# Attention streamed between the matmuls of a dense layer: pooled scores moved to columns of their own, into one insertion with the local scores, one slot later

## The chip, the cores and the metric

The kernel runs on one core of a Trainium2 chip. The engines are PE (TensorE, matmul), DVE (VectorE), ACT (ScalarE), POOL (GpSimd) and SP, which issues most of the DMAs. Each has its own instruction queue and runs it in order; semaphores tie them together. The metric is the time of one execution on the device in microseconds (us); lower is better. The median of three runs of the kernel before is 809.03 us (808.3 to 810.23).

## The reference, what matters

```python
# q, k, v: (4 batches, 8 heads, 576 positions, 64), fp32
q_d = q.reshape(B, H, 144, 4, 64).mean(axis=3)        # likewise k_d, v_d
out_d = softmax(scale * q_d @ k_d.T) @ v_d            # pooled attention, 144 x 144
out_up = np.repeat(out_d, 4, axis=2)
mask = abs(i - j) < 4                                 # local attention, a band of 7 keys
out_local = softmax(where(mask, scale * q @ k.T, -1e9)) @ v
x = (out_up + out_local) as (2304 tokens, 512)
h = x @ w_in;  x = (h * clip(h + 3, 0, 6) / 6) @ w_out          # d_ff 2048
h = max(x @ w1, x @ w2, x @ w3);  out = h @ w_out2              # d_ff 768
```

## The kernel before, in words

Attention is done for two heads at a time, a *pair*; there are 16 pairs, four to a batch (`PAIRS` = 4). Pairs 0 to 3 are done in a prologue, before the dense layers, with their instructions in an order written by hand. Pairs 4 to 15 are the *streamed* pairs: their instructions are put between the matmuls of the first dense layer, which makes PE the engine that has work all the time.

The first dense layer runs over 5 chunks of tokens (512 wide, the last one 256) and 16 slices of d_ff: 80 steps. Every product is made of three matmuls on high and low parts (`three`, L686 to L690). In step s, PE issues, in this order: `hidden(s + 1)`, the 12 matmuls of the first product for the next step; the even slot 2s; `add_out(s)`, the 12 matmuls of the second product; the odd slot 2s + 1. The hidden value goes through ACT (`gate_relu`, L1100), DVE (`gate`, L1384), ACT (`gate_high`, L1106) and DVE (`gate_low`, L1391); `add_out` waits for the last of them. `hidden(s)` waits until `gate(s - 1)` has emptied the one bank that it writes.

A *slot* is the place at which each engine puts in its part of a streamed pair (`attend`). `FIRST` (L145) gives the slot in which a pair starts: 0, 7, 14 and 21 for pairs 4 to 7, and 30, 38, 46 and so on to 86 for pairs 8 to 15. Pairs 5 and 7 so start in an odd slot, the others in an even one. `STAGES` (L146) gives how many slots later each stage comes:

- stage 0: PE transposes q and k (`turn_q`, `turn_k`), ACT copies them out (`copy_q`, `copy_k`, which count `s_cqk`), DVE sums them by fours (`pool_qk`), POOL sums v (`sum_v`).
- stage 1: PE makes the local scores (`scores_local`, L745, 20 products of 64 x 64, shown as 40 instructions) in columns 0 to 319 of the two banks `ba` and `bb`. DVE adds the mask (L1265), takes the maximum (L1273) and subtracts it (L1280).
- stage 2: PE makes the pooled scores (`scores_down`, L762, four products of 72 x 144, shown as 8 instructions) in columns 0 to 287 of the same two banks, once the mask has been added, that is once the local scores have been read. ACT takes the exponentials (`exp_local` L1024, `exp_down` L1033), DVE the pooled maximum (`max_down` L1309) and the local sum and its inverse (L1317 to L1323), POOL multiplies the local part (`norm_local`, L623).
- stage 2 plus one slot: DVE makes the inverse of the pooled sums (`inverse_down`, L1329, L1331), and POOL multiplies the pooled part by it (`norm_down`, L633).
- stage 3 (slot 5): PE transposes the local part (`turn_local`, L775) and then the pooled part (`turn_down`, L789), which waits for `norm_down`.
- stage 4 (slot 6): PE multiplies with v (L800, L823), and DVE adds both parts up into x (`put_x`, L1347).

In the first chunk the weights are split as well: ACT copies slice s + 3 (`high_w1`, L1072) right after `gate_high(s + 1)` and before the odd slot, and POOL subtracts (`low_w1`, L641). POOL's order in step s is: even slot 2s, `low_w1(s + 3)`, odd slot 2s + 1. The last slice, 15, is split in step 12. In steps 0 and 1 PE has no `hidden` of its own, since the prologue has done it; so nothing lies between slots 1 and 2 there.

DVE's order in step s is: `gate(s + 1)`, slot 2s, `gate_low(s + 1)`, slot 2s + 1. ACT's is: `gate_relu(s + 1)`, slot 2s, `gate_high(s + 1)`, `high_w1(s + 3)`, slot 2s + 1.

Of the kernel before, what the change touches and what calls it, by code (L numbers as in the profile page):

```python
# [7 lines left out]
ACT = mybir.ActivationFunctionType  # L8
# [53 lines left out]
def attention_moe_kernel(  # L62
# [18 lines left out]
    PAIRS = H // 2  # L81
# [8 lines left out]
    KW = 64  # L90
    QW = 58
    NT = 10
    TPH = NT // 2
# [7 lines left out]
    def tile_of(h, x, t):  # L101

        upper = (t + h) % 2
        return upper * LOWER[h] + 2 * (t // 2) + x
# [12 lines left out]
    SD = S // FACTOR  # L117
    DT = SD // 2
# [24 lines left out]

    FIRST = {4: 0, 5: 7, 6: 14, 7: 21, 8: 30, 9: 38, 10: 46, 11: 54, 12: 62, 13: 70, 14: 78, 15: 86}  # L145
    STAGES = (0, 1, 2, 5, 6)  # L146

    def at_slot(slot):

        return [(n, slot - a) for n, a in FIRST.items() if 0 <= slot - a <= STAGES[4]]  # L150

# [7 lines left out]
    def splits_of(slot):  # L159
        found = [EARLY[slot]] if slot in EARLY else []  # L160
        late = [(n // PAIRS, n // PAIRS, n % PAIRS) for n, a in FIRST.items() if slot == a + STAGES[4]]
        return found, late
# [56 lines left out]
    with ExitStack() as ctx:  # L219
# [4 lines left out]
        def sem(name):  # L224
            return ctx.enter_context(nc.semaphore(name))
# [61 lines left out]
        def tiles(n):  # L287
            return work_b if n == 1 else work_c if n == 2 else work_a
# [44 lines left out]
        s_cqk = sem("s_cqk")  # L333
        s_pool = sem("s_pool")
        s_sl = sem("s_sl")
        s_madd = sem("s_madd")
# [8 lines left out]
        s_dmax = sem("s_dmax")  # L345
# [218 lines left out]
        def _(pool):  # L564
# [35 lines left out]
            def sum_v(n):  # L600
                to, t = land(n), tiles(n)

                pool.wait_ge(to.s_v4, 32 * turn_of(n))
                g.tensor_tensor(to.v4[:, :, :, 0:2, :].rearrange("r t h j d -> r (t h) (j d)"),
                                to.v4[:, :, :, 0:2, :].rearrange("r t h j d -> r (t h) (j d)"),
                                to.v4[:, :, :, 2:4, :].rearrange("r t h j d -> r (t h) (j d)"),
                                ALU.add).then_inc(s_vpart, 1)
                pool.wait_ge(s_vpart, n + 1)
                if before(n) >= 0:

                    pool.wait_ge(s_pvd, before(n) + 1)
                g.tensor_tensor(t.vd[:].rearrange("r t (h d) -> r (t h) d", h=2),
                                to.v4[:, :, :, 0, :].rearrange("r t h d -> r (t h) d"),
                                to.v4[:, :, :, 1, :].rearrange("r t h d -> r (t h) d"),
                                ALU.add).then_inc(s_vd, 1)
# [30 lines left out]
            def attend(slot):  # L646
                for n, i in at_slot(slot):
                    if i == STAGES[0]:
                        sum_v(n)
                    if i == STAGES[2]:  # L650
                        norm_local(n)
                    if i == STAGES[2] + 1:
                        norm_down(n)
# [29 lines left out]
        def _(pe):  # L683
            mm = nc.tensor.matmul
# [41 lines left out]
            def scores_local(n):  # L726
                t = tiles(n)

                pe.wait_ge(s_cqk, 4 * n + 4)
                if n < PAIRS:  # L730

                    pe.wait_ge(s_mb, 1)
                    pe.wait_ge(s_idb, 1)
                    for x in range(2):
                        for h, dst in enumerate((t.ba, t.bb)):
                            rows = slice(h * KW, (h + 1) * KW)
                            mm(dst[x * KW:(x + 1) * KW, 0:TPH * KW], identb[rows, rows],
                               maskb[rows, x].rearrange("p t w -> p (t w)"), start=True, stop=False,
                               skip_group_check=True)
                for i in range(TPH):  # L740
                    for x in range(2):
                        for h, dst in enumerate((t.ba, t.bb)):
                            a = QW * tile_of(h, x, i)
                            rows = slice(h * D, (h + 1) * D)
                            mine = mm(dst[x * KW:(x + 1) * KW, i * KW:(i + 1) * KW], t.qT[rows, a:a + KW],  # L745
                                      t.kT[rows, a:a + KW], start=n >= PAIRS, stop=True, skip_group_check=True)
                mine.then_inc(s_sl, 1)

            def scores_down(n):
                t = tiles(n)  # L750

                pe.wait_ge(s_pool, 2 * n + 2)

                if n < PAIRS:
                    pe.wait_ge(s_lsub, n + 1)
                else:
                    pe.wait_ge(s_madd, 2 * (n - PAIRS) + 2)
                for i in range(2):
                    for h, dst in enumerate((t.ba, t.bb)):  # L760
                        rows = slice(h * D, (h + 1) * D)
                        mine = mm(dst[0:DT, i * SD:(i + 1) * SD], t.qd[rows, i * DT:(i + 1) * DT],  # L762
                                  t.kd[rows, :], start=True, stop=True)
                mine.then_inc(s_sd, 1)

            def turn_local(n):
# [61 lines left out]
            def attend(slot):  # L828
                for n, i in at_slot(slot):
                    if i == STAGES[0]:  # L830
                        turn_q(n)
                        turn_k(n)
                    if i == STAGES[1]:
                        scores_local(n)
                    if i == STAGES[2]:
                        scores_down(n)
                    if i == STAGES[3]:
                        turn_local(n)
                        turn_down(n)
                    if i == STAGES[4]:  # L840
                        values_down(n)
                        values_local(n)
# [157 lines left out]
        def _(act):  # L1000
            fn = nc.scalar.activation
# [24 lines left out]
            def exp_down(n):  # L1026
                t = tiles(n)

                act.wait_ge(s_dmax, 2 * n + 2)
                for h, src in enumerate((t.ba, t.bb)):  # L1030
                    for i in range(2):
                        at = 2 * h + i
                        mine = fn(t.dp[:, h, i, :], src[0:DT, i * SD:(i + 1) * SD], ACT.Exp,  # L1033
                                  bias=t.dnm[:, at:at + 1], accum_out=t.dsum[:, at, 0:1])
                mine.then_inc(s_dexp, 1)

# [209 lines left out]
        def _(dve):  # L1246
            vec = nc.vector
# [56 lines left out]
            def max_down(n):  # L1304
                t = tiles(n)

                dve.wait_ge(s_sd, n + 1)
                for h, src in enumerate((t.ba, t.bb)):
                    vec.tensor_reduce(t.dnm[:, 2 * h:2 * h + 2],  # L1309
                                      src[0:DT, 0:2 * SD].rearrange("p (t w) -> p t w", w=SD),  # L1310
                                      AX, ALU.max, negate=True).then_inc(s_dmax, 1)

            def inverse_local(n):
# [96 lines left out]
            for t in (work_a, work_b, work_c):  # L1410
# [4 lines left out]
                mine = vec.memset(t.qT[:, S:], 0.0)  # L1415
# [97 lines left out]
```

## Time and profile before

| | |
|---|---|
| median of three runs | 809.03 us |
| the profiled execution, its own time | 810.8 us |
| its span, first to last instruction | 809.0 us |
| PE matmul, busy | 793.4 us, 98% of the span |
| DVE, ACT, POOL, busy | 314.1, 277.3, 164.1 us |
| mean granted TensorE clock | 0.998 |
| the chain that ended last, share on PE | 93% |

How to read it: the two pieces of work that set the time are the matmuls themselves and the moments at which PE has none to issue. A row of the timeline is one group of instructions: its start, its length, the engine, line and operation, and in square brackets how long the engine was idle before it. Matmuls overlap in the pipeline, so the distance between two starts tells more than a length: undisturbed, the matmuls of the dense layer start about 0.23 us apart. The granted clock is at its upper level, 2.4 GHz, in all of the stretches that matter here.

### The profile page before, as it was taken

What the parts mean: (1) busy time and instruction counts of PE and PEld (TensorE: products, weight loads), DVE (VectorE), ACT (ScalarE), POOL (GpSimd) and SP (SyncE); (2) the same over time, 40 slices, a digit from 0 to 9 for tenths busy, and PEclk for the clock granted to TensorE, in tenths of its full rate; (3) what the DMA queues carried; (4) which work ended last, traced back from release to release, by engine and by line L of the source; (5) the groups of instructions that cost most, each with busy time, mean ns of one, the idle gap of its engine ahead of it and who ended that gap; (6) DMA issues with size and microseconds to landing.
All of it is one profiled execution on the core that took longest, in us unless ns stands there. A gap on an engine that the chain in (4) does not pass through costs nothing.

```text
span 809.0 us, 12700 instructions
## 1 busy us (share of the span) xinstructions
PE 793.4 (98%) x5344; PEld 659.0 (81%) x5344; DVE 314.1 (39%) x602; ACT 277.3 (34%) x619; POOL 164.1 (20%) x196
## 2 busy tenths in 40 slices
PE   7889999999999999999999999999999999999998
PEld 5667877888787878788888899888888888888897
DVE  5864556355444554553323334232123123112211
ACT  4745555343343434433223256221112112111111
POOL 7855756221022102210000048100000000000000
PEclk9999999999999999999999999999999999999999
DMA  8982412221211321110200066100110020010010
GB/s 176 207 260 69 113 48 61 57 79 39 62 39 32 103 62 32 30 32 30 76 1 0 1 196 188 61 0 1 53 52 1 36 70 0 14 66 0 14 40 27
DMA packets 93477, 49.06 MB, mean 61 GB/s; under 512 B 61164, under 2 KB 84204, under 8 KB 93420
## 3 DMA queue, kind: packets, MB, share of 16 engines
q1 hardware_dynamic: 90740, 47.36, 21.3%
q10 hardware_dynamic: 2680, 0.89, 0.6%
q8 instruction: 42, 0.69, 0.4%
q14 instruction: 15, 0.12, 0.1%
HBM read 38.79 MB, written 9.44 MB: 60 GB/s over the span
## 4 chain that ended last, share of the span: by engine, by line
PE 93%; POOL 2%; DVE 2%; ACT 1%; DMA 1%; SPq 1%; issue 1%; DVEq 0%; POOLq 0%
PE bank L688 29%; PE bank L690 28%; PE bank L689 28%; PE bank L823 1%; PE bank L800 1%; PE bank L745 1%; PE bank L789 1%; PE bank L762 1%; DMA k_nat_c<-in_k_dram 1%; PE bank L775 1%; POOL w L641 1%; PE bank L707 1%; POOL dp_a L633 1%; PE bank L717 1%; SPq L415 0%
## 5 line engine op out<-in xcount | busy, mean ns | idle before, releaser
L688 PE MATMUL bank<-xs,w 128*128 128x512 f32 (+1 forms) x680 | 253.5, 373 | 1.1 <-DVE xs L1356 1.0
L689 PE MATMUL bank<-xs,w 128*128 128x512 f32 (+1 forms) x680 | 250.5, 368 | 0.0
L690 PE MATMUL bank<-xs,w 128*128 128x512 f32 (+1 forms) x680 | 250.4, 368 | 0.0
L688 PEld LDWEIGHTS bank<-xs,w 128*128 128x128 f32 x680 | 128.4, 189 | 23.4 <-POOL w L641 1.4
L690 PEld LDWEIGHTS bank<-xs,w 128*128 128x128 f32 x680 | 128.3, 189 | 21.7
L689 PEld LDWEIGHTS bank<-xs,w 128*128 128x128 f32 x680 | 128.4, 189 | 20.4
L688 PE MATMUL bank<-gs,w 128*128 128x512 f32 (+1 forms) x320 | 121.6, 380 | 0.0
L1384 DVE SCALAR_TENSOR_TENSOR rg<-rg,bank 128x512 f32<-128x512 f32 (+1 forms) x80 | 50.7, 634 | 177.3 <-ACT rg L1100 177.3
L689 PE MATMUL bank<-gs,w 128*128 128x512 f32 (+1 forms) x320 | 118.1, 369 | 0.0
L690 PE MATMUL bank<-gs,w 128*128 128x512 f32 (+1 forms) x320 | 118.0, 369 | 0.0
L1100 ACT ACTIVATE rg<-bank,half 128x512 f32<-128x512 f32 (+1 forms) x80 | 51.6, 646 | 177.8 <-PE bank L690 177.8
L1391 DVE TENSOR_TENSOR gs<-rg,gs 128x512 fp32r<-128x512 f32 (+1 forms) x80 | 61.6, 770 | 39.2 <-ACT gs L1106 39.1
L1474 DVE TENSOR_TENSOR hm<-hm,bank 128x512 f32<-128x512 f32 (+1 forms) x30 | 19.0, 635 | 136.9 <-ACT hm L1215 136.9
L688 PEld LDWEIGHTS bank<-gs,w 128*128 128x128 f32 x320 | 60.3, 188 | 12.0 <-issue 1.9
L690 PEld LDWEIGHTS bank<-gs,w 128*128 128x128 f32 x320 | 60.3, 189 | 10.5
L689 PEld LDWEIGHTS bank<-gs,w 128*128 128x128 f32 x320 | 60.4, 189 | 8.9
L1215 ACT ACTIVATE hm<-bank 128x512 f32<-128x512 f32 (+1 forms) x30 | 16.7, 555 | 140.1 <-PE bank L690 140.1
L1106 ACT ACTIVATE gs<-rg 128x512 fp32r<-128x512 f32 (+1 forms) x80 | 47.3, 591 | 31.3 <-DVE rg L1384 31.3
L641 POOL TENSOR_TENSOR w<-w_raw,w 128x256 fp32r<-128x256 f32 x64 | 47.2, 768 | 28.4 <-ACT w L1072 28.4
L678 POOL TENSOR_TENSOR w<-w_raw,w 128x1024 fp32r<-128x1024 f32 x12 | 28.9, 2411 | 116.3 <-ACT w L1128 116.3
L1479 DVE TENSOR_TENSOR hs<-hm,hs 128x512 fp32r<-128x512 f32 (+1 forms) x30 | 19.2, 639 | 79.4 <-ACT hs L1223 79.4
L623 POOL TENSOR_TENSOR lp_a<-lp_a,linv_a 128x320 f32<-128x320 f32 x28 | 20.2, 741 | 145.8 <-DVE linv_a L1323 145.8
(211 smaller groups left out, 822.5 us busy)
## 6 DMA issues: line engine op xcount, KB each, us to landing
w_raw<-in_moe_w_out_dram SPq DMA_DIRECT2D x22, 256.0 KB, 4.8
w_raw<-in_moe_w_dram SPq DMA_DIRECT2D x18, 256.0 KB, 3.2
out_dram<-o_sb SPq DMA_DIRECT2D x18, 256.0 KB, 2.0
w_raw<-in_moe_w_in_dram SPq DMA_DIRECT2D x16, 256.0 KB, 3.9
x_scratch<-y SPq DMA_DIRECT2D x4, 1024.0 KB, 4.8
xr<-x_scratch SPq DMA_DIRECT2D x4, 1024.0 KB, 6.4
q_nat_a<-in_q_dram SPq DMA_DIRECT2D x26, 144.0 KB, 2.8
v_a<-in_v_dram SPq DMA_DIRECT2D x24, 144.0 KB
```

Source lines behind the costliest of these rows:

```text
L623: mine = g.tensor_tensor(lp[:, a:b], lp[:, a:b], t.linv[:, a:b].unsqueeze(2).to_broadcast([P, b - a, KW]), ALU.mult)
L641: mine = g.tensor_tensor(w1[:, f, 1, 2 * i:2 * i + 2], w1_raw[f][:, 2 * i:2 * i + 2], w1[:, f, 0, 2 * i:2 * i + 2].bitcast(F32), ALU.subtract)
L678: g.tensor_tensor(w2[:, m, 1], w2_raw[m][:], w2[:, m, 0].bitcast(F32), ALU.subtract).then_inc(s_w2, 1)
L688: mm(dst, w[0], m[0], start=start, stop=False, skip_group_check=True)
L689: mm(dst, w[0], m[1], start=False, stop=False, skip_group_check=True)
L690: return mm(dst, w[1], m[0], start=False, stop=stop, skip_group_check=True)
L1100: fn(gated(s), hidden_bank(s)[:, 0:n], ACT.Relu, bias=half[:, 0:1], scale=1.0 / 6.0).then_inc(s_relu, 1)
L1106: fn(gs[:, s % 2, 0, 0:n], gated(s), ACT.Copy).then_inc(s_gh, 1)
L1384: vec.scalar_tensor_tensor(out=gated(s), in0=gated(s), scalar=1.0, in1=hidden_bank(s)[:, 0:n], op0=ALU.min, op1=ALU.mult).then_inc(s_g, 1)
L1391: vec.tensor_tensor(gs[:, s % 2, 1, 0:n], gated(s), gs[:, s % 2, 0, 0:n].bitcast(F32), ALU.subtract).then_inc(s_gl, 1)
L1474: vec.tensor_tensor(got, got, bank[HBANK[f % 2][1]][:, 0:n], ALU.max).then_inc(s_m1, 1)
L1479: vec.tensor_tensor(hs[:, f, 1, 0:n], got, hs[:, f, 0, 0:n].bitcast(F32), ALU.subtract).then_inc(s_hl, 1)
```

## The change

`STAGES` goes from (0, 1, 2, 5, 6) to (0, 2, 3, 5, 6). In a streamed pair nothing is done in slot 1 any more. In slot 2 PE makes first the pooled scores and then the local scores; the pooled ones get columns that the local ones do not use, by the new function `pooled`: two of the four products go to a third bank (`bc`), one to `bb` and one to `ba` from column 320 on. `scores_down` no longer waits for the mask to be added. The work of DVE on the local scores moves to slot 2; the exponentials, `max_down`, `inverse_local` and `norm_local` move to slot 3; `inverse_down` and `norm_down` move to slot 4. The transposes stay in slot 5. `max_down` has three reductions in place of two. For the pairs of the prologue everything stays as it was.

```diff
-    STAGES = (0, 1, 2, 5, 6)
+    STAGES = (0, 2, 3, 5, 6)
+
+    def pooled(n, t, at):
+        if n < PAIRS:
+            return (t.ba, t.bb)[at // 2][0:DT, at % 2 * SD:(at % 2 + 1) * SD]
+        if at < 2:
+            return t.bc[0:DT, at * SD:(at + 1) * SD]
+        return (t.bb, t.ba)[at - 2][0:DT, TPH * KW:TPH * KW + SD]
...
# scores_down, PE
                 if n < PAIRS:
                     pe.wait_ge(s_lsub, n + 1)
                 else:
-                    pe.wait_ge(s_madd, 2 * (n - PAIRS) + 2)
+                    pe.wait_ge(s_cqk, 4 * n + 4)
                 for i in range(2):
-                    for h, dst in enumerate((t.ba, t.bb)):
+                    for h in range(2):
                         rows = slice(h * D, (h + 1) * D)
-                        mine = mm(dst[0:DT, i * SD:(i + 1) * SD], t.qd[rows, i * DT:(i + 1) * DT],
-                                  t.kd[rows, :], start=True, stop=True)
+                        mine = mm(pooled(n, t, 2 * h + i), t.qd[rows, i * DT:(i + 1) * DT],
+                                  t.kd[rows, :], start=True, stop=True, skip_group_check=True)
...
# attend, PE
                     if i == STAGES[1]:
+                        scores_down(n)
                         scores_local(n)
-                    if i == STAGES[2]:
-                        scores_down(n)
...
# exp_down, ACT
-                act.wait_ge(s_dmax, 2 * n + 2)
+                act.wait_ge(s_dmax, 2 * n + 2 + max(0, n - PAIRS + 1))
...
-                        mine = fn(t.dp[:, h, i, :], src[0:DT, i * SD:(i + 1) * SD], ACT.Exp,
+                        mine = fn(t.dp[:, h, i, :], pooled(n, t, at), ACT.Exp,
...
# max_down, DVE
+                parts = ((t.ba, 0, 0, 2), (t.bb, 0, 2, 4))
+                if n >= PAIRS:
+                    parts = ((t.bc, 0, 0, 2), (t.bb, TPH * KW, 2, 3), (t.ba, TPH * KW, 3, 4))
+                for src, first, a, b in parts:
+                    vec.tensor_reduce(t.dnm[:, a:b],
+                                      src[0:DT, first:first + (b - a) * SD].rearrange("p (t w) -> p t w", w=SD),
                                       AX, ALU.max, negate=True).then_inc(s_dmax, 1)
```

## Rows read from the trace of the kernel before

**Rows 1.** The page, busy time of each engine (share of the span, instructions).

```profile
PE 793.4 (98%) x5344; PEld 659.0 (81%) x5344; DVE 314.1 (39%) x602; ACT 277.3 (34%) x619; POOL 164.1 (20%) x196
```

**Rows 2.** Who waited for whom: total us, times, longest us.

```profile
PE bank L789 <- POOL dp_a L633: 1.6, 3, 0.8
PE bank L762 <- DVE lp_a L1265: 1.1, 1, 1.1
```

**Rows 3.** Timeline of PE, pair 9 (start, length, group).

```profile
188.24 0.39 PE L690 MATMUL bank<-gs,w 128*128 128x512 f32 x1
188.56 0.81 PE L745 MATMUL bank<-kT_a,qT_a 64*64 64x64 f32 x40
189.30 0.50 PE L688 MATMUL bank<-xs,w 128*128 128x512 f32 x1
...
191.93 0.39 PE L690 MATMUL bank<-xs,w 128*128 128x512 f32 x1
192.25 0.71 PE L762 MATMUL bank<-kd_a,qd_a 64*72 64x144 f32 x8
192.89 0.50 PE L688 MATMUL bank<-gs,w 128*128 128x512 f32 x1
...
195.74 0.39 PE L688 MATMUL bank<-xs,w 128*128 128x512 f32 x1
...
198.24 0.39 PE L690 MATMUL bank<-xs,w 128*128 128x512 f32 x1
...
201.19 0.71 PE L775 MATMUL bank<-ident,lp_a 128*128 128x128 f32 x5
201.73 0.67 PE L789 MATMUL bank<-ident,dp_a 72*72 72x72 f32 x8
```

**Rows 4.** Timeline of DVE and ACT, pair 9.

```profile
189.44 0.89 DVE L1265 TENSOR_TENSOR lp_a<-bank,mask 128x320 f32<-128x320 f32 x2 [0.83 <-PE bank L745]
...
191.22 0.82 DVE L1280 TENSOR_TENSOR lp_a<-lp_a,lnm_a 128x640 f32<-128x640 f32 x1
...
192.35 0.69 ACT L1100 ACTIVATE rg<-bank,half 128x512 f32<-128x512 f32 x1 [4.67 <-PE bank L690]
...
193.68 0.81 DVE L1309 TENSOR_REDUCE dnm_a<-bank 72x2 f32<-72x288 f32 x2
...
195.25 0.17 DVE L1321 TENSOR_REDUCE leps_a<-lsum_a 128x10 f32<-128x20 f32 x1
...
195.46 0.22 DVE L1323 RECIPROCAL linv_a<-leps_a 128x10 f32<-128x10 f32 x1
```

**Rows 5.** The page's group of gate_low on DVE.

```profile
L1391 DVE TENSOR_TENSOR gs<-rg,gs 128x512 fp32r<-128x512 f32 (+1 forms) x80 | 61.6, 770 | 39.2 <-ACT gs L1106 39.1
```

**Rows 6.** Timeline, pair 5, from the pooled maximum to norm_down.

```profile
85.81 0.81 DVE L1309 TENSOR_REDUCE dnm_a<-bank 72x2 f32<-72x288 f32 x2
...
88.10 0.69 ACT L1100 ACTIVATE rg<-bank,half 128x512 f32<-128x512 f32 x1
...
89.86 1.74 POOL L633 TENSOR_TENSOR dp_a<-dp_a,dinv_a 72x288 f32<-72x288 f32 x2 [0.58 <-DVE dinv_a L1331]
```

**Rows 7.** Line L633, norm_down (ns minimum/median/maximum).

```profile
L633 POOL TENSOR_TENSOR dp_a<-dp_a,dinv_a x28: 658/665/1118, 18.2 to 363.8; 72x288 f32<-72x288 f32 x28
```

**Rows 8.** Timeline, pair 4, norm_down behind low_w1.

```profile
60.52 0.81 DVE L1309 TENSOR_REDUCE dnm_a<-bank 72x2 f32<-72x288 f32 x2
...
64.47 2.84 POOL L641 TENSOR_TENSOR w<-w_raw,w 128x256 fp32r<-128x256 f32 x4 [0.47 <-ACT w L1072]
67.26 1.74 POOL L633 TENSOR_TENSOR dp_a<-dp_a,dinv_a 72x288 f32<-72x288 f32 x2
...
67.50 0.71 PE L775 MATMUL bank<-ident,lp_a 128*128 128x128 f32 x5
69.06 0.69 PE L789 MATMUL bank<-ident,dp_a 72*72 72x72 f32 x8 [0.85 <-POOL dp_a L633]
```

**Rows 9.** Timeline, pair 6, the start of turn_down.

```profile
119.15 0.70 PE L789 MATMUL bank<-ident,dp_a 72*72 72x72 f32 x8 [0.31 <-POOL dp_a L633]
```

More of the change, by code:

```diff
@@ L1027, in exp_down @@
                 t = tiles(n)
-                act.wait_ge(s_dmax, 2 * n + 2)
-                for h, src in enumerate((t.ba, t.bb)):
+                act.wait_ge(s_dmax, 2 * n + 2 + max(0, n - PAIRS + 1))
+                for h in range(2):
                     for i in range(2):
                         at = 2 * h + i
-                        mine = fn(t.dp[:, h, i, :], src[0:DT, i * SD:(i + 1) * SD], ACT.Exp,
+                        mine = fn(t.dp[:, h, i, :], pooled(n, t, at), ACT.Exp,
                                   bias=t.dnm[:, at:at + 1], accum_out=t.dsum[:, at, 0:1])
@@ L1307, in max_down @@
                 dve.wait_ge(s_sd, n + 1)
-                for h, src in enumerate((t.ba, t.bb)):
-                    vec.tensor_reduce(t.dnm[:, 2 * h:2 * h + 2],
-                                      src[0:DT, 0:2 * SD].rearrange("p (t w) -> p t w", w=SD),
+                parts = ((t.ba, 0, 0, 2), (t.bb, 0, 2, 4))
[4 more added lines that the diff above has]
+                                      src[0:DT, first:first + (b - a) * SD].rearrange("p (t w) -> p t w", w=SD),
                                       AX, ALU.max, negate=True).then_inc(s_dmax, 1)
```

## The prediction

> **What bounds the kernel now.** I read the page first: PE is busy for 98% of the span [rows 1]. Then the waits of PE: in the streamed pairs it waits for three things only, three times for POOL's `norm_down` (one of the three is in the prologue), and once, in pair 4, for the mask [rows 2]. So the time is the sum of what PE issues, and any wait that PE gets more of goes straight onto the time; nothing later can win it back. Then the timeline of PE around one pair, to price an insertion [rows 3], and those of DVE, ACT and POOL, to see how late the products of that pair arrive at slot 5 [rows 4 to 8]. The reader should see in these that the transposes of slot 5 now find everything ready in most pairs, and by how much.
>
> **The price of an insertion.** Undisturbed, a block of 12 matmuls goes from its first start to its last in 198.24 - 195.74 = 2.50 us, and 0.22 us lie between the last start and the next first. With the local scores ahead it is 189.30 - 188.24 = 1.06 from last to first, and the block takes 191.93 - 189.30 = 2.63. So this insertion costs 1.06 - 0.22 + 0.13 = 0.97. The pooled scores cost 192.89 - 191.93 - 0.22 + 0.13 = 0.87. Of each, 0.10 is entering (0.32 in place of 0.22) and 0.13 is the slower block behind; the instructions themselves are 0.74 and 0.64 [rows 3]. One insertion with both costs 0.10 + 0.64 + 0.74 + 0.13 = 1.61. That saves 0.23 us a pair. Bounds: 0.0, if entering the second kind of product inside the insertion costs as much as entering from outside and leaving, and 0.23. I take 0.23, because the row of the pooled scores gives 0.64 with a change of shape behind it as well.
>
 No row before has exactly this boundary in a streamed pair. If it cost the whole 0.23, the sum below would be 2.5 us higher.
>
> **Pair 4.** Slots 1 and 2 lie next to each other on PE there, and the wait for the mask goes: 1.1 us [rows 2]. Its start is not doubled, so I count nothing more than 0.1 for the gap around it: -1.2. At slot 5 it waits 69.06 - 67.50 - 0.54 = 1.02 now, where 0.54 is the undisturbed distance 201.73 - 201.19 [rows 3, 8]. That wait was made by `low_w1`, which no longer stands ahead of `norm_down`; but the chain is a slot later, and the wait will be about as long. Taken: the same, between 0.5 less and 0.5 more.
>
> **Pairs 8 to 15 (even start, no weights to split).** Let t = 0 be the start of the last matmul of `hidden(s + 1)` ahead of slot 2.
>
> - PE: pooled scores at 0.32, local scores at 0.96, `add_out(s)` from 1.70 to its last start 4.33, `hidden(s + 2)` 4.55 to 7.05, `add_out(s + 1)` 7.27 to 9.77, `turn_local` at 10.00, and `turn_down` would start at 10.54.
> - DVE can start on the local scores 189.44 - 188.56 = 0.88 after their start: 1.84. Mask to end of subtraction is 191.22 + 0.82 - 189.44 = 2.60: 4.44 [rows 3, 4]. Then `gate_low`, 0.77 [rows 5]: `max_down` starts at about 5.05, after the usual overlap of about 0.08 at either end.
> - `max_down` is three reductions. The bounds of the third are 0 (the columns are the same in all) and 0.37, the distance between the two of now (0.81 - 0.44). From 288 columns in 0.44 and 20 in 0.17 [rows 4], and 0.81 for the two in a row, a reduction of 144 is about 0.30, so the three take some 0.08 more than the two. I take 0.08.
> - From the start of `max_down` to the next `gate_relu` on ACT, when ACT is the one that holds it, are 88.10 - 85.81 = 2.29 [rows 6]: 5.05 + 2.29 + 0.08 = 7.42. PE holds it until 7.05 + 0.42 = 7.47 (0.42 is 192.35 - 191.93 [rows 3, 4]). So it starts at 7.47, and the chain of scores before it has only 0.05 us to spare.
> - `gate` and then `inverse_down` follow on DVE, since `inverse_down` now stands in slot 4, behind `gate(s + 2)`. In pair 5 of now exactly this order is seen: from `gate_relu` at 88.10 to the end of `norm_down` at 89.86 + 1.74 = 91.60 are 3.50 us [rows 6]. So it ends at 10.97.
> - PE starts 0.06 after POOL's end (69.00 to 69.06 [rows 8]): 11.03 in place of 10.54. PE waits 0.49 us, in each of 8 pairs, where it now waits for nothing.
>
> `norm_down` takes 1.74 in that order and 2 x 0.665 where DVE leaves it alone; single ones go up to 1.118 [rows 7]. With 1.30 the wait would be 0.05 only. The Trainium skill (SBUF — State Buffer, SBUF: two separate sides) has GpSimd and a VectorE operation with two SBUF inputs lock each other out for a whole instruction. The trace agrees: 1.118 against 0.665 us, and `gate_low`, which has two such inputs, comes 0.3 us behind `norm_down` in this order. By the rule the wait is 0.49 and not 0.05.
>
> Net: 8 x (0.49 - 0.23) = +2.1 us.
>
> **Pair 6 (even, with weights to split).** `gate_low` meets `low_w1` on POOL, as in pair 5 of now, and takes up to 0.5 longer; ACT then holds `gate_relu`, at about 7.9, and the wait is about 0.9. It is now 0.31 of idle time plus the 0.17 that pair 4 shows between idle time and real delay (1.02 against 0.85): 0.48 [rows 8, 9]. Net: 0.9 - 0.48 - 0.23 = +0.2.
>
> **Pairs 5 and 7 (odd start, with weights to split).** Here slot 3 is even and slot 4 odd, so `norm_down` moves from ahead of `low_w1` to behind it, in POOL's queue, and `low_w1(8)` (pair 7: `low_w1(15)`, the last) itself waits for ACT to get through `exp_down`, `gate_high` and `high_w1`. With t = 0 at the last matmul of `add_out` ahead of slot 2:
>
> - `hidden` 1.70 to 4.33; `gate_relu` at 4.75, `gate` at 5.47; `max_down` behind it at 6.08.
> - From the start of `max_down` to the start of `low_w1`, over `exp_down`, `gate_high` and `high_w1`, are 64.47 - 60.52 = 3.95 in pair 4 [rows 8], plus 0.08: 10.11.
> - `low_w1` holds POOL for 67.26 - 64.47 = 2.79: `norm_down` starts at 12.90. DVE has nothing with two SBUF inputs to do then, since its next `gate_low` waits behind the transposes: 1.30, ends at 14.20; PE at 14.26.
> - PE's `turn_down` would start at 10.54. It waits 3.7 us.
>
> Net: 2 x (3.7 - 0.23) = +6.9 us. Bounds of one wait: 2.8 (if `norm_local` and the weights slip by a third of that) and 4.2 (`norm_down` at 1.74).
>
> **Sum.** -1.2 + 2.1 + 0.2 + 6.9 = +8.0 us. On the profiled execution (span 809.0, own time 810.8) this is 818.8; that one is 1.8 above the median of the runs, so on the median it is 817.0. Everything else costs nothing or hides: nothing moves on SP's queue and no DMA is added; the third reduction is on DVE, 39% busy [rows 1], and counts only through the chain above.
>
> **The rivals.**
>
> 1. *The even pairs have no wait, the odd ones do.* If `gate_low` comes late enough, `norm_down` takes 1.30. For it: most single ones take 0.665 [rows 7]. Against it: pair 5 of now. 8 x (0.05 - 0.23) + 0.2 - 1.2 + 6.9 = +4.5: 813.5.
> 2. *The even chain is late by itself.* Only 0.05 us are to spare ahead of `gate_relu`. If the third reduction costs 0.37 and the merged insertion saves nothing, the even pairs wait 0.3 longer (9 pairs, +2.6) and 11 pairs lose the 0.23 (+2.5): 822.
> 3. *The other side: one insertion fewer is all that counts.* POOL and DVE keep up, `norm_down` ends before PE gets to `turn_down`, and what is left is 11 x 0.23 + 1.2 = 3.7 us less: 805.3. The place is slot 5, and the deciding point is `norm_down` ending before t = 10.5. For it: pairs 5 and 7 to 15 don't wait there now, and the mask's wait goes. Against it: in pairs 8 to 15 the order of DVE's queue puts the end at 10.97, and in pairs 5 and 7 it would have to come 3.7 us earlier than POOL's queue lets it.
> 4. *Nothing to be seen:* wait and saving cancel, which needs the odd pairs' wait to be a third of what I have: 809.
>
> **How the numbers follow.** Forecast 0.72, rival 1 0.10, rival 2 0.10, rival 3 0.05, rival 4 0.03. Faster or slower by 0.2% (1.6 us) is about what a measurement can tell from no change: faster 0.05, same 0.03, slower 0.92. The range has the bounds of the odd pairs (-1.8, +1.0), of the saving (+2.5), of pair 4 (0.5 either way) and reaches to rival 1 and near to rival 2: 813.0 to 821.0.
>
> **What would show it.** Right: a wait of PE at L789 for POOL's L633 of about 3.7 us in pairs 5 and 7, with L641 directly ahead of L633 on POOL, and of about 0.5 in pairs 8 to 15, with L633 at 1.74 for two; no wait at L762 in pair 4; 1.70 us from the last matmul ahead of slot 2 to the first one behind. Wrong: L789 without a wait in the odd pairs, or L633 ahead of L641 there; L745 taking clearly more than 0.74 behind L762; `gate_relu` starting later than 0.42 after the last matmul in pairs 8 to 15.

## The result, and the profile after

The changed kernel takes 822.25 us, median of 4 runs (821.21 to 823.96); the kernel before, beside it, 809.63 us (808.3 to 812.01). The ratio is 1.0161, 95% interval 1.0145 to 1.0178: slower, by 12.6 us. The forecast was +8.0 us, 817.0 us, range 813 to 821. The direction and the waits are as forecast; the size is not. In one execution of `e1_order` (982.03 us) and one of `e9_early_w11` (851.59 us) the granted clock was lower throughout, 0.75 and 0.88; they are left out of all the ratios.

The profiled run of the changed kernel took 821.21 us, its span is 819.4. First the page, busy time of each engine: PE is busy 3.8 us longer than before with the same 5344 instructions [rows 1], a first sign that some of them got slower; the rest of the 10.4 us by which the span grew is idle time.

```profile
PE 797.2 (97%) x5344; PEld 662.5 (81%) x5344; DVE 310.3 (38%) x614; ACT 278.5 (34%) x619; POOL 166.1 (20%) x196
```

Then the waits of PE (total us, times, longest), to be held against [rows 2]:

```profile
PE bank L799 <- POOL dp_a L642: 12.7, 13, 3.5
```

L799 is `turn_down` (L789 before) and L642 `norm_down` (L633 before). From pair 4 on PE waits for it 12 times, before twice (pairs 4 and 6, 1.2 us in all). The wait for the mask in pair 4 is gone.

**Where the time came in.** I count from the first transposes of one streamed pair (q_nat_a, L707 before, L716 after) to those of the next. This leaves out the prologue, whose end moves between 49.8 and 53.4 us from execution to execution and blurs any comparison of spans. "Late" is how much later `turn_down` starts behind `turn_local` than the undisturbed 0.54 us [rows 3].

| pair | step before | step after | difference | forecast | late before | late after |
|---|---|---|---|---|---|---|
| 4 | 24.32 | 23.99 | -0.33 | -1.2 | 1.02 | 1.76 |
| 5 | 24.80 | 29.82 | +5.02 | +3.47 | 0 | 3.62 |
| 6 | 25.30 | 26.16 | +0.86 | +0.2 | 0.48 | 1.35 |
| 7 | 30.24 | 35.27 | +5.03 | +3.47 | 0 | 3.63 |
| 8 to 15, each | 27.51 | 27.83 | +0.32 | +0.26 | 0 | 0.49 |

The sum is +13.1 us, and from the first transposes of pair 4 to the end of the span it is 769.6 - 756.5 = 13.1 us as well. So all of it lies in these rows.

Pair 8, the timeline of PE around slots 2 and 5 of the changed kernel:

```profile
171.30 0.39 PE L699 MATMUL bank<-xs,w 128*128 128x512 f32 x1
171.62 0.71 PE L772 MATMUL bank<-kd_a,qd_a 64*72 64x144 f32 x8
172.26 0.81 PE L754 MATMUL bank<-kT_a,qT_a 64*64 64x64 f32 x40
173.00 0.50 PE L697 MATMUL bank<-gs,w 128*128 128x512 f32 x1
...
181.32 0.71 PE L785 MATMUL bank<-ident,lp_a 128*128 128x128 f32 x5
182.35 0.44 PE L799 MATMUL bank<-ident,dp_a 72*72 72x72 f32 x4 [0.33 <-POOL dp_a L642]
```

With t = 0 at 171.30, the block behind the insertion starts at 1.70 (forecast 1.70), `turn_local` at 10.02 (10.00) and `turn_down` at 11.05 (11.03). The reader should notice that the idle time in brackets, 0.33, is less than the delay: 182.35 - 181.32 - 0.54 = 0.49. The same pair on DVE, ACT and POOL:

```profile
176.26 0.88 DVE L1323 TENSOR_REDUCE dnm_a<-bank 72x2 f32<-72x288 f32 x3
...
178.79 0.69 ACT L1110 ACTIVATE rg<-bank,half 128x512 f32<-128x512 f32 x1
...
180.56 1.73 POOL L642 TENSOR_TENSOR dp_a<-dp_a,dinv_a 72x288 f32<-72x288 f32 x2 [0.76 <-DVE dinv_a L1345]
```

`max_down` starts at t = 4.96 (forecast 5.05), `gate_relu` at 7.49 (7.47), `norm_down` ends at 10.99 (10.97). Pair 5, POOL and then PE:

```profile
88.30 1.41 POOL L632 TENSOR_TENSOR lp_a<-lp_a,linv_a 128x320 f32<-128x320 f32 x2 [4.61 <-DVE linv_a L1337]
90.16 2.78 POOL L650 TENSOR_TENSOR w<-w_raw,w 128x256 fp32r<-128x256 f32 x4 [0.46 <-ACT w L1082]
92.89 1.28 POOL L642 TENSOR_TENSOR dp_a<-dp_a,dinv_a 72x288 f32<-72x288 f32 x2
...
90.07 0.71 PE L785 MATMUL bank<-ident,lp_a 128*128 128x128 f32 x5
94.23 0.70 PE L799 MATMUL bank<-ident,dp_a 72*72 72x72 f32 x8 [3.46 <-POOL dp_a L642]
...
95.28 0.40 PE L699 MATMUL bank<-gs,w 128*128 128x512 f32 x1
95.51 0.55 PE L697 MATMUL bank<-gs,w 128*128 128x512 f32 x1
95.85 0.63 PE L698 MATMUL bank<-gs,w 128*128 128x512 f32 x1
96.28 0.63 PE L699 MATMUL bank<-gs,w 128*128 128x512 f32 x1
```

The order on POOL is the one forecast, `norm_local`, `low_w1`, `norm_down`, and the wait of PE too: `turn_down` 3.62 us late (forecast 3.7). But look at the starts of the matmuls behind it. To 95.51 they are 0.23 apart, from 95.85 on 0.43. That is what the forecast didn't have. The windows of the two odd pairs, of pair 7 the one behind the wait only (PE, PEld, DVE, ACT and POOL busy with counts, then the granted clock, the DMA share and GB/s):

```profile
90.30:94.20 3.90, 0.48 (x5) 0.24 (x3) 0.88 (x3) 1.14 (x2) 3.88 (x6) 1.00 0.00 0
94.20:95.50 1.30, 1.27 (x11) 1.15 (x12) 0.00 (x0) 0.53 (x3) 0.00 (x0) 1.00 0.00 0
95.50:98.80 3.30, 3.30 (x9) 2.56 (x8) 0.69 (x1) 1.80 (x4) 1.43 (x3) 0.52 0.00 0
...
150.20:153.40 3.20, 3.18 (x13) 2.73 (x14) 0.55 (x1) 1.38 (x4) 1.18 (x1) 0.50 0.02 5
```

After 3.5 us in which PE did nothing, the granted clock is at half (1.2 GHz) for some 3.3 us of full work. In pair 5 the fall comes 1.3 us after PE is at work again. My theory: this costs 1.55 us in each of the two pairs, 3.1 of the 5.1 us by which the forecast falls short. Rivals: that the wait itself is worth more than its length (buffers that come free later, DMAs that start later), or that something else in those pairs, the weights' split beside it, slows the matmuls down.

### The profile page after: what moved, and what is told of

The parts are those of the page before. It is cut to its first block, busy times and chain, and to the rows that moved or that the text cites. A ratio compares the mean times of both kernels' runs of the same rounds, so it can differ in the third digit from the quotient of the medians.

```text
span 819.4 us, 12712 instructions
## 1 busy us (share of the span) xinstructions
PE 797.2 (97%) x5344; PEld 662.5 (81%) x5344; DVE 310.3 (38%) x614; ACT 278.5 (34%) x619; POOL 166.1 (20%) x196
## 4 chain that ended last, share of the span: by engine, by line
PE 86%; POOL 5%; DVE 4%; ACT 2%; DMA 1%; issue 1%; SPq 1%; DVEq 0%; ACTq 0%; POOLq 0%
PE bank L697 27%; PE bank L699 26%; PE bank L698 26%; POOL dp_a L642 3%; PE bank L833 1%; PE bank L799 1%; DVE rg L1398 1%; ACT rg L1110 1%; PE bank L810 1%; POOL w L650 1%; PE bank L772 1%; DMA k_nat_c<-in_k_dram 1%; PE bank L754 1%; ACT dp_a L1043 1%; PE bank L716 1%
## 5 line engine op out<-in xcount | busy, mean ns | idle before, releaser
L1405 DVE TENSOR_TENSOR gs<-rg,gs 128x512 fp32r<-128x512 f32 (+1 forms) x80 | 59.1, 739 | 37.2 <-ACT gs L1116 37.1
L699 PEld LDWEIGHTS bank<-gs,w 128*128 128x128 f32 x320 | 61.1, 191 | 10.9
L697 PEld LDWEIGHTS bank<-gs,w 128*128 128x128 f32 x320 | 61.0, 191 | 10.5
L698 PEld LDWEIGHTS bank<-gs,w 128*128 128x128 f32 x320 | 61.1, 191 | 9.3
```

What stands on the lines that cost most here:

```text
L697: mm(dst, w[0], m[0], start=start, stop=False, skip_group_check=True)
L698: mm(dst, w[0], m[1], start=False, stop=False, skip_group_check=True)
L699: return mm(dst, w[1], m[0], start=False, stop=stop, skip_group_check=True)
L1405: vec.tensor_tensor(gs[:, s % 2, 1, 0:n], gated(s), gs[:, s % 2, 0, 0:n].bitcast(F32), ALU.subtract).then_inc(s_gl, 1)
```

## The experiments

All are edits of the changed kernel, but for `d1_behind`, which is one of the kernel before. "From first transposes" is the span less the start of the streamed part, held against 756.5 of the kernel before.

| kernel | ratio to before, interval | from first transposes | steps 4, 5, 6, 7, 8 | late 4, 5, 6, 7, 8 |
|---|---|---|---|---|
| a1_again | 1.0162 [1.0146, 1.0179] | 770.8 | 23.99, 29.84, 26.00, 36.41, 27.83 | 1.76, 3.63, 1.35, 3.62, 0.49 |
| e1_order | 1.0086 [1.0059, 1.0113] | 761.7 | 23.97, 25.96, 25.97, 31.39, 27.83 | 1.75, 1.33, 1.35, 1.33, 0.49 |
| e2_warm | 1.0143 [1.0126, 1.0160] | 766.6 | 23.99, 28.26, 25.97, 34.04, 27.83 | 1.75, 3.64, 1.35, 3.64, 0.49 |
| e10_warm457 | 1.0118 [1.0102, 1.0133] | 766.3 | 23.98, 28.27, 25.97, 33.68, 27.84 | 1.76, 3.64, 1.34, 3.62, 0.49 |
| d1_behind | 1.0045 [1.0029, 1.0061] | 759.5 | 24.31, 26.26, 25.30, 31.70, 27.52 | 1.01, 1.44, 0.47, 1.44, 0 |
| e5_early | 0.9980 [0.9966, 0.9995] | 754.4 | 22.91, 25.47, 24.92, 30.91, 27.30 | 0.70, 0.85, 0.30, 0.84, 0 |
| e3_merge1 | 1.0059 [1.0041, 1.0077] | 759.6 | 25.01, 24.64, 26.04, 30.08, 28.03 | 1.02, 0, 1.04, 0, 0 |
| e4_apart | 1.0277 [1.0247, 1.0307] | 778.0 | 23.99, 31.01, 26.49, 36.70, 28.51 | 1.75, 3.62, 1.51, 3.62, 0.97 |
| e8_w11 | 1.0177 [1.0149, 1.0204] | 770.2 | 25.61, 29.87, 25.11, 35.27, 27.83 | 1.75, 3.62, 0.50, 3.62, 0.49 |
| e9_early_w11 | 0.9972 [0.9957, 0.9987] | 754.1 | 22.93, 25.46, 24.59, 30.90, 27.31 | 0.70, 0.84, 0.01, 0.84, 0 |

**e1_order**: in the two odd pairs POOL puts the weights' split behind `norm_down`.

```diff
-                if s + 3 < F1:
+                if s + 3 < F1 and s not in (5, 12):
...
+                if s in (5, 12):
+                    low_w1(s + 3)
```

> The changed kernel, with POOL doing low_w1 of steps 5 and 12 behind the odd slot in place of ahead of it, so that norm_down of pairs 5 and 7 no longer stands behind it. Theory (POOL's order makes the wait of 3.6 us, and the granted clock falls behind so long a wait): PE's extra delay at turn_down falls from 3.62 to about 1.4 us in both pairs (inverse_down on DVE ends 10.5 us after the last matmul ahead of slot 2, norm_down takes 1.3), the clock stays at its upper level, and the time falls by 2 x (2.2 + 1.55) = 7.5 us, to about 5 us above the kernel before. Rival A (the slow stretch has nothing to do with the length of the wait, any wait in these pairs brings it): only 4.5 us less. Rival B (norm_down is held by something else than low_w1, such as inverse_down behind ACT): less than 1 us less.

POOL's timeline around pair 5:

```profile
91.89 1.29 POOL L642 TENSOR_TENSOR dp_a<-dp_a,dinv_a 72x288 f32<-72x288 f32 x2 [0.91 <-DVE dinv_a L1347]
93.14 2.82 POOL L650 TENSOR_TENSOR w<-w_raw,w 128x256 fp32r<-128x256 f32 x4
```

PE's waits from 45 us on; L801 is `turn_down`:

```profile
PE bank L801 <- POOL dp_a L642: 7.6, 12, 1.5
```

The longest is 1.5 now. The delay falls from 3.62 to 1.33 and the two steps from 29.82 and 35.27 to 25.96 and 31.39. In pair 5 that is 3.86 us, where the shorter wait accounts for 2.29: the other 1.57 is more than the wait. So POOL's queue makes the wait, and the wait brings something that is not its length. The total is 7.9 us below the changed kernel by the trace (769.6 - 761.7). The timed runs scatter widely here (814.58, 815.66 and 818.81), so I go by the steps.

**e2_warm**: 36 matmuls of nobody's use ahead of the wait in pairs 5 and 7, so that PE waits but is not idle.

```diff
+                    if n in (5, 7):
+                        for _ in range(36):
+                            mm(t.bb[:, 288:496], idle[:, 0:P], idle[:, 0:208], start=True, stop=True, skip_group_check=True)
```

> The changed kernel, with 36 bf16 matmuls of 208 columns into columns of bank bb that nobody uses, ahead of the wait of turn_down in pairs 5 and 7: PE is busy for about 3.1 of the 3.6 us for which it waits. Theory (the clock falls because PE was idle): the wait stays as it is, the granted clock stays at its upper level behind it, and the time falls by 2 x 1.55 = 3.1 us, to about 9.7 us above the kernel before. Rival (the slow stretch is not PE's idle time, but for example the restart of the two-pass work or what the other engines do): time unchanged at about 12.6 above before, and the clock at 0.5 for 3.3 us behind both waits. If the matmuls last longer than the wait, the time would rise by what is over.

The delay stays at 3.64, the step of pair 5 falls to 28.26: 1.56 less than in the changed kernel with the same wait, and 28.26 - 24.80 = 3.46 above before, the forecast's 3.47. In pair 7 it is 34.04, with a granted clock of 1.00, 1.23 less than in the changed kernel. The gain would be like that of pair 5 but for a wait of 0.33 us for a DMA at the start of pair 7, which the changed kernel does not have there:

```profile
132.37 0.37 PEld L726 LDWEIGHTS bank<-ident,k_nat_a 96*128 96x128 f32 x4 [0.33 <-DMA k_nat_a<-in_k_dram]
```

Without it pair 7 gains 1.56 too. In the timed runs the interval of the ratio, 1.0126 to 1.0160, overlaps that of the changed kernel, 1.0145 to 1.0178. Therefore I ran it again, with more such matmuls, beside the changed kernel on the same chip.

**a1_again** is the changed kernel, unchanged.

> The changed kernel itself once more, beside the next one on the same chip, to have its median against that. Theory: 12.5 to 13.1 us above before, as the trace of it has it (13.1 us between the first transposes of pair 4 and the end).

Its median is 13.2 us above that of the kernel before beside it. In its profiled execution it is 14.3, and pair 7 takes 36.41 in place of 35.27 with the same delay: 1.1 us more, for which the windows below give the reason.

**e10_warm457**: matmuls of nobody's use in pairs 4 (18 of them), 5 and 7 (38).

```diff
+                    if n in (4, 5, 7):
+                        for _ in range(18 if n == 4 else 38):
+                            mm(t.bb[:, 288:496], idle[:, 0:P], idle[:, 0:208], start=True, stop=True, skip_group_check=True)
```

> The changed kernel with PE kept busy by bf16 matmuls ahead of turn_down in pairs 4, 5 and 7 (18, 38 and 38 of them; 3.3 of 3.6 us in the long ones), to settle in timed runs what the slow clock costs; the earlier run with pairs 5 and 7 alone showed 3.0 us in its trace, but a median only 1.5 us nearer to before. Theory: the delays stay at 1.75, 3.62 and 3.62, the clock at its upper level; 3.1 us less than the changed kernel run beside it, a little more where that one falls in pair 4 too. Rival (the time of the slow stretch is won back elsewhere): less than 1 us between the two medians.

PE of `e10_warm457` in pair 5:

```profile
91.77 3.55 PE L794 MATMUL bank<-ident 128*128 128x208 bf16 x38
95.40 0.70 PE L802 MATMUL bank<-ident,dp_a 72*72 72x72 f32 x8
```

Its windows behind the waits of pairs 5 and 7 (columns as above):

```profile
95.40:99.00 3.60, 3.60 (x22) 2.81 (x24) 0.69 (x1) 2.33 (x5) 0.46 (x1) 1.00 0.00 0
151.00:155.00 4.00, 4.00 (x60) 3.04 (x59) 0.94 (x2) 1.03 (x3) 0.73 (x1) 1.00 0.04 10
```

The same two places in `a1_again`:

```profile
95.00:99.00 4.00, 3.76 (x15) 3.16 (x16) 0.69 (x1) 2.33 (x5) 0.51 (x2) 0.57 0.00 0
151.00:155.00 4.00, 3.93 (x15) 3.35 (x16) 0.69 (x1) 1.39 (x4) 1.24 (x2) 0.50 0.01 4
...
151.07:156.90 5.83, 5.83 (x20) 4.70 (x20) 0.69 (x1) 1.39 (x4) 1.17 (x1) 0.50 0.01 3
```

Granted clock 1.00 against 0.57 and 0.50, with the same delay in front (3.64 and 3.62 against 3.63 and 3.62). The steps are 1.57 and 2.73 us shorter than in `a1_again`, and the median goes from 823.09 to 819.38 us; the intervals of the two ratios do not overlap. That is 3.7 us, more than the 3.1 expected, because the stretch in pair 7 of `a1_again` is longer than those of the changed kernel. The delays, and with them the weights' split and the buffers' release, are alike in both. This shows that the idle time itself makes the slow stretch, and it gives its price: 1.57 to 2.73 us each. The price goes with the length of the stretch: 1.57 for 3.4 us of work at half clock (pair 5), 2.73 for 5.83 (pair 7), a bit less than half of it in both.

**d1_behind**: in the kernel before, `norm_down` of pairs 5 and 7 is put behind `low_w1` in POOL's queue; the scores stay where they were.

```diff
-                    if i == STAGES[2] + 1:
+                    if i == STAGES[2] + 1 and n not in (5, 7):
                         norm_down(n)
...
+                if s in (5, 12):
+                    norm_down({5: 5, 12: 7}[s])
```

> The kernel before, with only norm_down of pairs 5 and 7 put behind low_w1 in POOL's queue, everything else as before, stages too: the same order in the queue as in the changed kernel, with one slot more of slack. Theory: low_w1(8) starts when high_w1(8) ends (91.1), takes 2.8, norm_down 1.3: turn_down starts 1.5 us late in both pairs, the clock does not fall (the changed kernel shows a delay of 1.8 us in pair 4 without a fall), and the time rises by 3 us over before. Rival A (every wait of more than a microsecond brings the slow clock): 6 us more than before. Rival B (the order of POOL's queue is not what counts): no change.

POOL's timeline around pair 5:

```profile
89.62 2.81 POOL L641 TENSOR_TENSOR w<-w_raw,w 128x256 fp32r<-128x256 f32 x4 [1.93 <-ACT w L1074]
92.39 1.29 POOL L633 TENSOR_TENSOR dp_a<-dp_a,dinv_a 72x288 f32<-72x288 f32 x2
```

The same order as in the changed kernel, but only 1.44 late, without a slow stretch, and 3.0 us in all. So the order alone does not make the 3.6, and neither do the later scores alone (1.33 in `e1_order`): it takes both. The scores that come a slot later push ACT's part of the weights, and with it `low_w1`, back too: it starts 0.1 us behind `turn_local` in the changed kernel (90.16 and 90.07), and 2.1 us ahead of it here (89.62 and 91.76).

**e5_early**: the changed kernel with `inverse_down` (DVE) and `norm_down` (POOL) back in slot 3.

```diff
-                    if i == STAGES[2] + 1:
+                    if i == STAGES[2]:
                         norm_down(n)
...
-                    if i == STAGES[2] + 1:
+                    if i == STAGES[2]:
                         inverse_down(n)
```

> The changed kernel, with inverse_down on DVE and norm_down on POOL put in slot 3, behind inverse_local and norm_local, in place of slot 4. Theory (it is not the later slot of the scores but the place of inverse_down behind gate(s + 2), and of norm_down behind low_w1, that makes PE wait): no wait at turn_down in pairs 8 to 15 (norm_down ends 9.9 us after the last matmul ahead of slot 2, turn_down would start at 10.5), about 0.6 in pairs 5 and 7 and no slow clock, about 0.8 in pair 4: 15 us less than the changed kernel, 2 to 3 us less than before. Rival (the chain of the scores itself is too long for its slots): waits of 0.3 us or more stay in pairs 8 to 15, or new waits of add_out for gate_low come up, and the time stays above before.

Pairs 8 to 15 now have no wait and take 27.30: 27.51 - 27.30 = 0.21 us is what one insertion fewer saves. Every delay in pairs 4 to 7 is 0.85 us or less, no slow stretch is seen behind any of them, and the kernel is slightly faster than before: from first transposes 2.1 us, ratio 0.9980, interval 0.9966 to 0.9995.

**e3_merge1**: both scores together in slot 1, where the local ones stood, so the insertion is merged and nothing is late.

```diff
-    STAGES = (0, 2, 3, 5, 6)
+    STAGES = (0, 1, 2, 5, 6)
```

> The changed kernel with STAGES back at (0, 1, 2, 5, 6): both kinds of scores in one insertion at slot 1, everything on the other engines at the slots of before. Theory (an insertion fewer saves 0.23 us of PE's own time, but the slot that it leaves is one in which the other engines had time): norm_down is in time in pairs 8 to 15, no wait at turn_down there; but slot 2 is then only two blocks of 12 matmuls long, and gate_low, which stands behind exp_down and inverse_local, ends 5.8 to 5.9 us after the last matmul ahead of slot 2, where add_out wants it at 5.4: a wait of 0.4 to 0.5 us for gate_low in each of pairs 8 to 15, and the step from pair to pair 27.7 us (27.51 before, 27.83 changed). Odd pairs 0.2 less than before; pair 6 and pair 4 0.6 more each. In all about 2.5 us above before. Rival (a merged insertion at slot 1 is free of waits): 27.28 us from pair to pair, and 3 us less than before.

The waits of PE's weight load, from 45 us on:

```profile
PEld bank L697 <- DVE gs L1405: 5.0, 8, 1.5
```

One of the eight, around the 199th us, on PE and DVE:

```profile
198.63 0.39 PE L699 MATMUL bank<-xs,w 128*128 128x512 f32 x1
199.10 0.50 PE L697 MATMUL bank<-gs,w 128*128 128x512 f32 x1
...
194.94 0.88 DVE L1323 TENSOR_REDUCE dnm_a<-bank 72x2 f32<-72x288 f32 x3
195.74 0.81 DVE L1331 TENSOR_REDUCE lsum_a<-lp_a 128x10 f32<-128x640 f32 x1
...
197.96 1.09 DVE L1405 TENSOR_TENSOR gs<-rg,gs 128x512 fp32r<-128x512 f32 x1 [0.95 <-ACT gs L1116]
```

`turn_down` is on time, but now the block after next waits for its gate: DVE's queue holds `max_down` and the sums ahead of `gate_low`, and `add_out`'s first matmul starts 0.47 us after its predecessor in place of 0.23. The steps of pairs 8 to 14 are 27.67 to 27.69, but for 28.0 in pairs 8 and 12, where PE waits for a copy on DVE (L1412) instead. As expected there is a loss, but it is larger: 3.1 us by the trace (759.6 - 756.5), 4.1 in the medians, in place of 2.5. Merging alone gives nothing back: 1.0059. Without the later slot the wait stands in another place.

**e4_apart**: pooled scores in slot 2 as in the changed kernel, but the local ones in slot 1 again: two insertions, everything else late (the mask waits for the pooled scores too).

```diff
+                    if i == 1:
+                        scores_local(n)
                     if i == STAGES[1]:
                         scores_down(n)
-                        scores_local(n)
...
+                dve.wait_ge(s_sd, n + 1)
```

> The changed kernel with the local scores made in slot 1, alone, and the pooled ones in slot 2, alone: two insertions as before, while the mask and all that follows stays in the later slots (DVE waits for both kinds of scores before it adds the mask). Theory (in pairs 8 to 15 norm_down hangs on gate(s + 2), which PE or ACT lets go 7.4 to 7.5 us after the last matmul ahead of slot 2, whatever the insertion holds): PE is 0.74 us earlier at turn_down and waits that much longer, 1.2 us in place of 0.49; the insertion on its own costs 0.23 more. The step from pair to pair is 27.83 + 0.69 + 0.23 - 0.0 = 28.7 us at most. Rival (the chain follows PE, so that the wait stays 0.49): 28.06 us. Rival (two insertions cost no more than one): 27.83 us with the wait at 0.49.

PE, POOL and ACT in pair 8:

```profile
186.99 0.71 PE L785 MATMUL bank<-ident,lp_a 128*128 128x128 f32 x5
188.49 0.69 PE L799 MATMUL bank<-ident,dp_a 72*72 72x72 f32 x8 [0.79 <-POOL dp_a L642]
...
186.70 1.74 POOL L642 TENSOR_TENSOR dp_a<-dp_a,dinv_a 72x288 f32<-72x288 f32 x2 [0.55 <-DVE dinv_a L1346]
...
184.94 0.68 ACT L1110 ACTIVATE rg<-bank,half 128x512 f32<-128x512 f32 x1
```

Pairs 8 to 15 are 0.97 late, 0.2 less than I expected (I had taken 0.77 us for `gate_low` where it takes 0.69, and ACT lets `gate_relu` go 7.21 us after the last matmul ahead, not 7.4). The step is 28.51, 0.68 over the changed kernel: 0.48 more wait and 0.20 for the second insertion. So the merged insertion hides some of the lateness; without it the change costs 2.8%. Part of that is longer slow stretches in pairs 5 and 7, with 5.5 and 6.1 us of work at half clock.

**e8_w11**: the changed kernel with the slice 11 of the weights split one step earlier on ACT and POOL, so that `low_w1` doesn't stand beside `gate_low` in pair 6.

```diff
-                if s + 3 < F1:
+                if s + 3 < F1 and s != 8:
...
+                if s == 7:
+                    low_w1(11)
...
+                if s == 7:
+                    high_w1(11)
```

> The changed kernel with slice 11 of the weights split one step earlier (step 7, on ACT and POOL), so that POOL is idle while DVE works on the local scores of pair 6. Theory (the delay of 1.35 us in pair 6 in place of 0.49 comes from low_w1 on POOL running beside DVE's subtraction and gate_low, 1.32 and 1.23 us in place of 0.82 and 0.69): these fall back, the delay at turn_down in pair 6 is 0.5 and the step from pair 6 to pair 7 is 25.1 us in place of 25.97 to 26.16; pair 4, where nothing is moved, keeps 1.75. Rival (the length of ACT's queue makes it): the delay stays above 1.2.

DVE in pair 6, first of the changed kernel, then of `e8_w11`:

```profile
113.69 1.32 DVE L1290 TENSOR_TENSOR lp_a<-lp_a,lnm_a 128x640 f32<-128x640 f32 x1
114.93 1.23 DVE L1405 TENSOR_TENSOR gs<-rg,gs 128x512 fp32r<-128x512 f32 x1
```

```profile
116.67 0.83 DVE L1294 TENSOR_TENSOR lp_a<-lp_a,lnm_a 128x640 f32<-128x640 f32 x1
117.41 0.68 DVE L1409 TENSOR_TENSOR gs<-rg,gs 128x512 fp32r<-128x512 f32 x1
```

The two operations with two operands in SBUF take 0.49 and 0.55 us longer while POOL splits weights. Without the split beside them pair 6 is 0.50 late, as pairs 8 to 15 are, and its step is 25.11. The gain does not reach the total, because in this execution pair 4 had a slow stretch that none of the five other executions with the same delay of 1.75 there had:

```profile
68.00:70.00 2.00, 2.00 (x9) 1.61 (x7) 0.00 (x0) 0.86 (x3) 2.00 (x4) 0.54 0.03 8
```

Its step is 25.61 where the others have 23.97 to 23.99.

**e9_early_w11**: both edits, `norm_down` and `inverse_down` in slot 3 and slice 11 a step earlier.

> The changed kernel with inverse_down and norm_down in slot 3 (the version whose time was below before) and slice 11 of the weights split one step earlier as well. Theory: steps of 27.30 us in pairs 8 to 15 as measured without the second edit, pair 6 without a delay (0.3 less), pairs 5 and 7 at 0.85: 2.4 us less than before, 0.3% faster. Rival (the gain seen was scatter of the runs): ratio to before 0.999 to 1.001.

807.0 us, median of the ten runs that count, beside 809.08 of the kernel before; ratio 0.9972, interval 0.9957 to 0.9987, which excludes the rival's 0.999. It beats both kernels, if by 0.3% only. Its gain over `e5_early` is not shown, as the two intervals overlap; only the step of pair 6 is shorter, by 0.3. POOL in pair 8:

```profile
170.29 1.29 POOL L642 TENSOR_TENSOR dp_a<-dp_a,dinv_a 72x288 f32<-72x288 f32 x2
```

`norm_down` runs at 1.29 for two here, 1.73 in the changed kernel: it is all but done (171.58) when the next `gate_low` starts on DVE (171.42).

## Why the prediction was right in kind and wrong in size

**The step that failed** is the price of the wait in the odd pairs: "PE's `turn_down` would start at 10.54. It waits 3.7 us. Net: 2 x (3.7 - 0.23) = +6.9 us." The wait is right (3.62 and 3.63). Pricing a wait of TensorE by its length alone was wrong; what comes behind it was put at nothing, without a reason. The two pairs cost 5.02 and 5.03, of which 1.56 and 1.59 (29.82 - 28.26 and 35.27 - 33.68) come from matmuls at half the clock. `e2_warm` and `e10_warm457` show it by taking the idle time away under an equal wait; `e1_order`, with a shorter wait, agrees. The bounds (2.8 and 4.2) were bounds of the wait, so they had no room for it.

The trace of before did show such a stretch, in the prologue, at a wait which the prediction does not count (windows first, columns as above, then PE's timeline):

```profile
31.00:35.00 4.00, 1.27 (x28) 0.94 (x21) 3.24 (x10) 2.57 (x5) 3.60 (x5) 1.00 0.99 266
35.00:38.00 3.00, 3.00 (x20) 2.33 (x18) 2.60 (x2) 3.00 (x13) 3.00 (x5) 0.53 1.11 212
```

```profile
34.69 0.76 PE L789 MATMUL bank<-ident,dp_c 72*72 72x72 f32 x8 [2.73 <-POOL dp_c L633]
```

PE waits 2.73 us for the same instruction, and the clock in the 3 us behind is 0.53. The forecast wait of 3.7 is longer than that, so the row gave reason to expect a fall. The Trainium skill (TensorE: Matmul & The Clock Gate, What's actually happening) has the clock fall to 1.2 GHz when the array is idle. The traces agree, with 0.50 to 0.57 behind the waits of 3.6.

**Pair 4** was to win 1.2 and won 0.33. The wait for the mask went, as forecast, but "the wait will be about as long" did not hold: it is 1.76 in place of 1.02, outside the 0.5 that I had allowed. `low_w1` doesn't stand ahead of `norm_down` any more, but beside `gate_low` and the subtraction on DVE (1.23 and 1.22 us where 0.69 and 0.83 are undisturbed). `e8_w11` shows this effect in pair 6; in pair 4 no run tests it.

**Pair 6** was to lose 0.2 and lost 0.86 (0.70 in `a1_again`). PE waits 0.17 us at its start (104.23) for the DMA that brings k, which `a1_again` does not show, so 0.7 is the change's part. That is still 0.5 too much. I had added the disturbance of `gate_low`, but not that of the subtraction ahead of it. `e8_w11` shows that both together are 0.85 us of the delay (1.35 to 0.50).

**Pairs 8 to 15** were right to 0.1 us in every term: insertion 1.70, `gate_relu` 7.49, `norm_down` 1.73, late 0.49. The net is 0.32 rather than 0.26, since one insertion fewer saves 0.21 (`e5_early`) and a wait of 0.49 costs 0.53 (27.83 - 27.30). That gives 0.5 us in all.

By terms, over the forecast of +8.0: slow stretches +3.1, pair 4 +0.9, pair 6 +0.7 (0.2 of it the wait for k), pairs 8 to 15 +0.5. This makes 13.2; measured in the trace 13.1, in the medians 12.6.

**Rivals.** Rival 1 (no wait in the even pairs) is out: `norm_down` takes 1.73 for two. Rival 2 is out: `gate_relu` starts when PE lets it, and the third reduction costs 0.07 (0.88 against 0.81). Its 822 us came true for another reason. Rival 3 didn't happen, but its mechanism is real: take the lateness away (`e5_early`, `e9_early_w11`), and one insertion fewer leaves 2.1 to 2.4 us. Rival 4's condition was worked out wrongly: with the odd pairs' wait at a third, 1.2 us, the same sum gives -1.2 + 2.1 + 0.2 + 2 x (1.2 - 0.23) = +3.0, and with no wait there at all still +0.6.

## What to carry to other kernels

Where TensorE is the bound, price a new wait in two parts: its length, and, once it gets to the length of waits behind which the trace already shows a lower granted clock, the slow stretch behind it. Look for such a wait in the trace of before, the prologue too. As an estimate from `a1_again` and `e10_warm457`, the slow stretch costs a bit less than half of the time that the work in it takes. When a step moves to a later slot, work out anew which instructions of other queues it is now behind and beside: here most of what was lost in pairs 5 and 7 came from POOL's split of the weights, which the change doesn't touch (with the split out of the way, 1.33 of the 3.62 us stay). And one insertion fewer is worth 0.2 us here, so a single microsecond of lateness eats five of them.

## What the runs showed of the hardware that I had not expected

- The clock can fall after work has begun again: in pair 5 PE starts at 94.23 and the matmuls are further apart from 95.51 on, for 3.4 us. It can also fall within the wait and stay down for longer: in pair 7 of `a1_again` it is down before PE starts at 151.07 (0.54 between 150.00 and 151.07), and then for 5.8 us of work; in `e4_apart` for 5.5 and 6.1 us.
- Delays of 1.51 us and less in the streamed pairs were never followed by a slow stretch here. Delays of 3.6 us always were, where PE had nothing else to do: eight of them, two each in the changed kernel, `a1_again`, `e4_apart` and `e8_w11`. With 1.75 us in pair 4 one of six executions had it (`e8_w11`). What decides in between stays open; I can't tell from these runs. It is not the length of a single wait alone. In the prologue of the changed kernel the clock fell at 20.5 us, where the longest waits of PE in the 5 us before were 0.90 and 0.48 (windows before and after the fall, columns as above, then PE's timeline):

```profile
17.00:20.50 3.50, 2.12 (x22) 1.47 (x20) 3.47 (x11) 1.02 (x4) 3.39 (x5) 1.00 0.84 206
20.50:23.90 3.40, 3.40 (x55) 2.64 (x56) 2.66 (x7) 2.86 (x12) 3.16 (x4) 0.50 0.71 161
```

```profile
18.57 0.77 PE L785 MATMUL bank<-ident,lp_a 128*128 128x128 f32 x5 [0.90 <-POOL lp_a L632]
```

- Two tile shapes directly behind each other in one insertion (64 by 72, then 64 by 64) cost no more than their own time: 172.26 - 171.62 = 0.64 and 173.00 - 172.26 = 0.74, the same as each alone [rows 3]. The Trainium skill (TensorEngine Tiling (Array Packing), Key Properties) has a change of mode drain TensorE; if it does here, the drain costs nothing that these rows can tell from none.
